# Later weight passes of a two-layer feed-forward kernel: who sums and rounds the first-layer weights, and where the second weights are fetched

## The reference

```python
def _moe_ref(x, w_in, w_out):            # first layer
    h = x @ w_in
    return ((h * (1.0 / (1.0 + np.exp(-h)))) @ w_out).astype(np.float32)

def _moe2_ref(x, w_in, w_out):           # second layer
    h = x @ w_in
    g = h * np.clip(h + 3.0, 0.0, 6.0) / 6.0
    return (g @ w_out).astype(np.float32)
```

## Time and profile before

| what | value |
|---|---|
| median of three runs | 1698.34 us |
| the profiled execution's own time | 1697.79 us |
| its span | 1696.0 us |
| TensorE busy | 1674.4 us, 99% |
| VectorE busy | 1043.5 us, 62% |
| ScalarE busy | 726.3 us, 43% |
| GpSimd busy | 354.2 us, 21% |
| granted TensorE clock, mean | 0.993 |

### The profile page before, as it was taken

One profiled execution on the slowest core, in us unless ns is written; L12 is line 12 of the kernel. 1 busy time (PEld: TensorE's weight loads), 2 busy tenths in 40 slices (PEclk: granted clock), 3 DMA queues, 4 the chain that ended last, 5 costly groups with the idle time before them and its releaser, 6 DMA issues.

```text
span 1696.0 us, 27977 instructions
## 1 busy us (share of the span) xinstructions
PE 1674.4 (99%) x11352; PEld 1504.7 (89%) x11352; DVE 1043.5 (62%) x1568; ACT 726.3 (43%) x1183; POOL 354.2 (21%) x443
## 2 busy tenths in 40 slices
PE   8899999999999999999999999999999999999999
PEld 7878988898899999999999899999998899999998
DVE  8856656756647555555557655555557766666664
ACT  4655555555545433333334434333335433333332
POOL 6665543644106300000006200000006200000000
PEclk8899999999999999999999999999999999999999
DMA  8333343433213322222224211111112322222221
GB/s 218 81 113 107 107 115 98 118 107 111 71 46 103 123 79 77 75 75 81 75 78 140 82 51 54 53 51 50 52 58 85 116 75 76 80 76 77 79 77 50
DMA packets 129840, 145.86 MB, mean 86 GB/s; under 512 B 47536, under 2 KB 74416, under 8 KB 129712
## 3 DMA queue, kind: packets, MB, share of 16 engines
q1 hardware_dynamic: 79968, 127.95, 23.1%
q10 hardware_dynamic: 49744, 16.13, 3.8%
HBM read 96.86 MB, written 47.19 MB: 85 GB/s over the span
## 4 chain that ended last, share of the span: by engine, by line
PE 93%; DVE 4%; ACT 1%; issue 1%; DMA 0%; POOL 0%; ACTq 0%; SPq 0%; DVEq 0%; POOLq 0%
PE zw L629 8%; PE zw L631 8%; PE zw L630 8%; PE acc L715 6%; PE xy L629 6%; PE xy L631 6%; PE xy L630 6%; PE acc L716 5%; PE acc L717 5%; PE acc L721 4%; PE acc L722 4%; PE acc L723 4%; PE att L722 4%; PE att L723 4%; PE att L721 4%; PE att L716 2%
## 5 line engine op out<-in xcount | busy, mean ns | idle before, releaser
L1232 DVE TENSOR_TENSOR g_lo<-g_raw,g_hi 128x1024 fp32r<-128x1024 f32 x144 | 196.1, 1364 | 9.1 <-ACT g_raw L932 9.1
L920 ACT COPY x_sum<-xy 128x256 f32<-128x256 f32 x144 | 52.4, 365 | 293.9 <-PE xy L631 293.7
L1197 DVE TENSOR_TENSOR x_sum<-xy,x_sum 128x256 f32<-128x256 f32 x144 | 60.6, 421 | 189.5 <-ACT x_sum L920 189.5
L629 PE MATMUL xy<-xr_hi,w1r_hi 128*128 128x256 f32 x576 | 166.2, 289 | 1.9 <-DVE x_sum L1197 1.9
L534 POOL TENSOR_TENSOR w_sum<-w_raw 128x256 f32<-128x256 f32 x16 | 16.6, 1035 | 712.2 <-DMA w_raw<-in_moe_w_in_dram 712.2
L631 PE MATMUL xy<-xr_hi,w1r_lo 128*128 128x256 f32 x576 | 163.4, 284 | 0.0
L630 PE MATMUL xy<-xr_lo,w1r_hi 128*128 128x256 f32 x576 | 163.4, 284 | 0.0
L715 PE MATMUL acc<-g_hi,w_hi 128*128 128x512 f32 x400 | 162.8, 407 | 0.0
L1221 DVE TENSOR_TENSOR g_raw<-zw,x_sum 128x512 f32<-128x512 f32 x144 | 99.1, 688 | 95.2 <-PE zw L631 95.2
L717 PE MATMUL acc<-g_hi,w_lo 128*128 128x512 f32 x400 | 156.4, 391 | 0.0
L716 PE MATMUL acc<-g_lo,w_hi 128*128 128x512 f32 x400 | 156.3, 391 | 0.0
(11 more groups left out here) (212 smaller groups left out, 4860.5 us busy)
## 6 DMA issues: line engine op xcount, KB each, us to landing
partial<-y_stage SPq DMA_DIRECT2D x72, 256.0 KB, 2.1
y_part<-partial SPq DMA_DIRECT2D x18, 1024.0 KB, 5.9
x_raw<-first_layer_t SPq DMA_DIRECT2D x18, 1024.0 KB, 7.7
x_raw<-attended_t SPq DMA_DIRECT2D x10, 1024.0 KB, 8.1
first_layer_t<-y_stage SPq DMA_DIRECT2D x36, 256.0 KB, 2.0
out_dram<-y_stage SPq DMA_DIRECT2D x36, 256.0 KB, 2.0
w_raw<-in_moe_w_in_dram SPq DMA_DIRECT2D x16, 512.0 KB, 4.2
kv_stage<-in_v_dram SPq DMA_DIRECT2D x56, 144.0 KB
```

The costliest lines, as they stand in the source:

```text
L629: nc.tensor.matmul(dst, s_hi[i], m_hi[i], start=first and i == 0, stop=False, skip_group_check=True)
L1232: nc.vector.tensor_tensor(g_lo[:, p], g_raw[:, p % 2], g_hi[:, p].bitcast(fp32), ALU.subtract)\
```

## The change

GpSimd no longer sums pair 3 of passes 1 to 3: VectorE does it, at place U + 14, with a semaphore of its own. ScalarE's roundings of the next pass's pairs move from chunks 5 and 6 to chunks 7 and 8 (places 6 and 7) and from U + 12 and U + 16 to U + 16 and U + 20; VectorE's last split moves from U + 21 to U + 22. The roundings of the second weights move from places 1 to 8 to the places in `W2_AT`. SyncE fetches f = 0 and 1 behind the first two stores, f = 2 and 3 behind the last two, and f = 4 to 7 behind the loads of the partials and of x.

```diff
-W1_ROUND_AT = [4, 5, U + 12, U + 16]
-W1_SPLIT_AT = [U + 18, U + 21]
+W1_ROUND_AT = [6, 7, U + 16, U + 20]
+W1_SUM_AT = U + 14
+W1_SPLIT_AT = [U + 18, U + 22]
+
+W2_AT = [1, 1, 2, 6, 7, U, U + 4, U + 8]
...
-                if ps and blk == 0:
-                    for f in range(4, NF):
-                        load_w2(ps, f)
                 if ps % 2:
                     load_part(s)
...
                 if blk == NB - 1 and ps + 1 < PASSES:
                     load_w1(ps + 1, 2)
                     load_w1(ps + 1, 3)
-                    for f in range(4):
-                        load_w2(ps + 1, f)
+                if ps and blk == 0:
+                    for f in range(4, NF):
+                        load_w2(ps, f)
                 for j in range(NK):
                     store_y(s, j)
+                    if blk == NB - 1 and ps + 1 < PASSES and j % 2:
+                        load_w2(ps + 1, j - 1)
+                        load_w2(ps + 1, j)
...
                 sums(ps, 2)
-                sums(ps, 3)
...
-                act.wait_ge(w1_summed, 4 * (ps * NPAIR + p) + 4)
+                if ps == 0:
+                    act.wait_ge(w1_summed, 4 * (p + 1))
+                elif p < 3:
+                    act.wait_ge(w1_summed, 4 * (NPAIR + 3 * (ps - 1) + p + 1))
+                else:
+                    act.wait_ge(w1_last_summed, 4 * ps)
...
-                    if ps and blk == 0 and 1 <= place <= NF:
-                        round_w2(ps, place - 1)
+                    for f in range(NF):
+                        if ps and blk == 0 and place == W2_AT[f]:
+                            round_w2(ps, f)
...
+            def sum_w1(ps, p):
+
+                n = 4 * (ps - 1)
+                raw, sums_ = w1_source(ps, p)
+                a11, a21, a12, a22 = w1_blocks(raw)
+                s3, s2, s4 = (sums_[:, i].rearrange("p (c f) -> p c f", c=2) for i in range(3))
+                dve.wait_ge(w1_loaded[p % 2], 16 * (2 * (ps - 1) + p // 2 + 1))
+                nc.vector.tensor_tensor(s3, a11, a21, ALU.subtract).then_inc(w1_last_summed, 1)
+                dve.wait_ge(w1_last_summed, n + 1)
+                nc.vector.tensor_tensor(a21, a21, a22, ALU.add).then_inc(w1_last_summed, 1)
+                dve.wait_ge(w1_last_summed, n + 2)
+                nc.vector.tensor_tensor(s2, a21, a11, ALU.subtract).then_inc(w1_last_summed, 1)
+                dve.wait_ge(w1_last_summed, n + 3)
+                nc.vector.tensor_tensor(s4, a12, s2, ALU.subtract).then_inc(w1_last_summed, 1)
...
+                    if blk == NB - 1 and ps + 1 < PASSES and place == W1_SUM_AT:
+                        sum_w1(ps + 1, NPAIR - 1)
                     if blk == NB - 1 and ps + 1 < PASSES and place in W1_SPLIT_AT:
                         split_w1(ps + 1, 2 + W1_SPLIT_AT.index(place))
```

More of the change, by code:

```diff
@@ L342, in build @@
         uh_done = sem("uh_done")
+        w1_last_summed = sem("w1_last_summed")
         g_split = sem("g_split")
@@ L524, in sums @@
             def sums(ps, p):
-                n = 4 * (ps * NPAIR + p)
+                n = 4 * (ps * NPAIR + p if ps == 0 else NPAIR + 3 * (ps - 1) + p)
                 raw, sums_ = w1_source(ps, p)
```

## The result

The changed kernel takes 1701.29 us, median of 20 runs (1699.27 to 1702.84), against 1698.29 us for the kernel before in 20 runs (1696.69 to 1699.57). The medians differ by 3.0 us; the ratio of all runs is 1.0016, with a 95% interval of 1.001 to 1.0021. That is slower by less than the 0.2% that I had called the limit, though the interval excludes no change. The forecast was 1701.5.

What follows compares the result with a forecast made beforehand. TensorE, busy 99% of the span, was taken as the bound, with only its stalls to win. Steps 9, 18, 26 and 27 (+1.1, +3.1, -1.8, +0.8) give +3.2 us: 1697.79 to 1701.0, median 1701.5, range 1696.3 to 1704.5.

Steps and rivals of the forecast that it cites:

- The stalls of before: Steps 18, 26 and 27 lost 1.8, 2.2 and 3.4 us; all would go but 0.4 in step 26.
- Turns between GpSimd and VectorE: Their SBUF instructions run one after the other: 15.1 us from T24.4 (us into step 17), x ending at T40.4.
- the stalls at b0: Stalls before chunk b0 of steps 9, 18 and 27: 1.0, 3.1 and 2.5 us, released by L1197.
- The four sums: Pair 3's sums on VectorE: 0.46 us each with the gap, 1.8 in all; nothing won on GpSimd.
- f = 7: Last second-weight tile, split late for the 26th unit of steps 18 and 27: stall 1.65 us, bounds 0 to 2.3.
- TensorE's clock: Rival, chance 0.15: after step 18's 3.1 us stall, 3.3 us at half speed lose 1.7, giving 1703.2.
- The sum: Step 9 +1.1, step 18 +3.1, step 26 -1.8, step 27 +0.8 us; together +3.2, median 1701.5.
- the lower bound: From 1701.5 down, without both f = 7 stalls (3.3) and with sums at 0.34 us (1.4): 1696.5.
- Late fetches: Fetches behind stores cost nothing; rival, chance 0.05: ScalarE waits at place 1, 1.3 us in three steps, 1705.4.

Runs made afterwards that it cites:

- e2_gpsimd_sums: Changed kernel with pair 3's four sums back on GpSimd, right behind pair 2's: 1706.52 us, ratio 1.0044.
- e6_w2_places: Kernel before with only the second weights rounded at the changed kernel's places (W2_AT): 1708.17 us, ratio 1.0054.
- e5_split_late: Changed kernel with pair 3's rounding and VectorE's split of it at U + 28, between second and third evacuations: 1694.92 us, ratio 0.9976.
- e1_rounds_back: Changed kernel with the roundings of the next pass's pairs 0 and 1 back in chunks 5 and 6: 1696.21 us, ratio 0.9985.
- e9_w2_and_fetch: Kernel before with W2_AT's rounding places and the fetches of f = 4 to 7 behind the loads of partials and x: 1697.15 us, ratio 0.999.
- e3_f7_early: Changed kernel with the last second-weight tile rounded at U + 5 instead of U + 8: 1698.63 us, ratio 0.9999.
- e10_changed_again: The changed kernel itself run once more for a second profile: 1699.37 us.
- e7_mixed: Changed kernel, roundings of pairs 0 and 1 in chunks 5 and 6 behind steps 8 and 17 only, last second-weight tile at U + 5: 1693.36 us, ratio 0.9972.
- e11_mixed_again: e7_mixed run once more for a second profile: 1693.55 us.
- e4_stores_first: Kernel before with only the fetches of f = 0 to 3 issued behind the first two and last two stores: 1696.71 us, ratio 0.999.

## Why the prediction was right

**The stalls of before.** Right. Step 26 was put at 42.4 and took 42.31; the stalls at b2 and b3 of steps 18 and 27 went.

**Turns between GpSimd and VectorE.** Right in mechanism. I had 15.1 us of turns from T24.4 on in step 17, then 0.3 of gaps and 0.6 for VectorE's last instruction. The trace has 15.1 us in all, from 913.31 (the end of the first L568, 910.39 + 2.92) to 928.42, and VectorE's last instruction is in it: L1319 started at 927.82. So the turns took 14.5, not 15.1, there were no gaps beside them, and they began 0.1 earlier. That is the mis-sized term: x ended at T39.4, not T40.4, and at T41.5, not T42.3, in step 26. Everything behind came about 1 us earlier, and the stalls at b0 were 0.4, 2.25 and 2.15 instead of 1.0, 3.1 and 2.5.

**The four sums.** 0.41 to 0.43 us each, 1.7 in all, for 1.8. That nothing was won on GpSimd, which I had written, is wrong: e2_gpsimd_sums shows 3.8 us. GpSimd "was idle by then" only because the sums were no longer there. It did not touch the forecast, which never needed that figure.

**f = 7.** Right in place and cause, 1.2 for 1.65.

**TensorE's clock.** A rival, with 0.15, for a stall of 3.1. It came with stalls of 2.25 and 2.15, in steps 18 and 27 in this profile; I had it for step 18 alone. The price was too high: 1.35 to 1.5 each, not 1.7. I had taken 3.3 us at half speed as half lost, but in these chunks the spacing of the matmuls goes only from 0.12 to 0.213 us. It nearly doubles, from 0.227 to 0.427, in the units behind the stall of 5.3 of e6_w2_places; step 9 there is 49.0 = 41.94 + 5.3 + 1.7. The Trainium skill, TensorE: Matmul & The Clock Gate, section "What's actually happening", has the slow clock as the idle state; the trace agrees that it follows idleness, and e5_split_late that it goes when the stall goes.

**The sum.** It met the median through two errors of opposite sign. The stalls were 0.5 (step 9) + 0.85 + 0.35 + 2 x 0.45 = 2.6 us smaller than forecast, and the clock, left out of the sum, gave 2.7 in this profile and half of that in the next. What holds is the direction and its cause, the turns, which e1_rounds_back confirms; that 1701.5 fits to 0.2 us is luck. A slip beside it: the terms of the lower bound, 3.3 and 1.4, give 1696.8, not 1696.5.

**Late fetches** cost nothing in the changed kernel, as said. In step 18 ScalarE did wait 3.0 us for f = 0, until 938.70 (T7.7; I had put its landing at 5.5); but TensorE was stalled until 938.81 by VectorE, and no wait of TensorE's followed from it. What I had said too lightly is that "SyncE's other moves wait for nothing that isn't done": e6_w2_places shows that the move of f = 4 to 7 is what keeps the later roundings from costing some 11 us (1708.17, a ratio of 1.0054, against 1697.15, 0.999, in e9_w2_and_fetch), with three half clocks among them.

## What to carry to other kernels

In the stretches seen here, the work of VectorE with two operands in SBUF and that of GpSimd add up as if on one engine (15 instructions in 14.5 us in step 17), so moving GpSimd work later in a step is only free if VectorE has no deadline there; count both queues' instructions from the last point where they were free. Work whose result is wanted late (here pair 3) belongs into the wait for a store, not ahead of the evacuations, since the next step's ring stands behind them. When places of work move, check every in-order queue whose next entry waits for them, and price a TensorE stall of 2.2 us as possibly 3.6.

## What the runs showed of the hardware that I had not expected

The half clock starts at shorter stalls than I had bound from the earlier trace rows, and not each time. Of eight stalls of 2.15 to 2.25 us at chunk b0 (changed kernel 2, e3_f7_early 2, e10_changed_again 2, e7_mixed 1, e11_mixed_again 1) five were followed by 3.4 us at the 1.2 GHz level and three were not. Of six stalls of 1.8 to 2.0 us (kernel before, e1_rounds_back, e2_gpsimd_sums, e4_stores_first, e6_w2_places, e9_w2_and_fetch) it followed one, a stall of 1.99 in step 26 of e6_w2_places, and not the one of 1.99 in the same step of the kernel before. The four of 2.6 us and more (2.9 and 3.97 in e2_gpsimd_sums, 5.3 and 2.6 in e6_w2_places) all had it. In e3_f7_early it began 1.2 and 1.7 us after the matmuls had resumed, in the other runs within 0.5. What decides in between was not tried.
